# Moving eighteen row scalings from VectorE to GpSimd at the end of an attention and mixture-of-experts kernel

## What is computed

```python
x = attention(q, k, v)                 # 2304 tokens x 512, chunks of 64
h = x @ w_in;  x = (h * clip(h + 3, 0, 6) / 6) @ w_out
noisy_logits = x @ w_gate + log1p(exp(x @ w_noise)) * noise
top2 = ...; top2_w = softmax over the two
out = zeros((2304, 512))
for e in range(8):
    for k in range(2):                 # tokens whose k-th choice is e
        out[mask] += top2_w[mask, k, None] * (relu(x[mask] @ w1[e]) @ w2[e])
```

## Time and profile before

| | us |
|---|---|
| median of three runs | 1018.02 |
| lowest and highest | 1017.66, 1019.82 |
| the profiled execution | 1018.02 |
| its span, first to last instruction | 1016.4 |
| TensorE busy | 988.8 (97%) |
| GpSimd busy | 479.7 (47%) |
| VectorE busy | 444.6 (44%) |
| TensorE's mean granted clock | 0.994 |

### The profile page before, as it was taken

The page is one execution under the profiler, slowest core; times in us unless marked ns, Lnnn a source line. Parts: engine busy times, 40 slices in busy tenths (PEclk is TensorE's granted clock), DMA queues, the critical chain, the costliest instruction groups (busy, mean ns, idle before and its releaser), DMA issues.

```text
span 1016.4 us, 18598 instructions
## 1 busy us (share of the span) xinstructions
PE 988.8 (97%) x5883; PEld 835.9 (82%) x5884; DVE 444.6 (44%) x848; ACT 340.9 (34%) x483; POOL 479.7 (47%) x743
## 2 busy tenths in 40 slices
PE   6999999999999999999999999999999999999997
PEld 6888988987988988988877878878787887888885
DVE  5454355344345445464454443334334333433334
ACT  3333333332343343332422333333333333333332
POOL 5994001100100200597463785848578584934344
PEclk9999999999999999999999999999999999999999
DMA  9832032132123120524366455656656565346629
GB/s 331 305 100 64 18 108 84 46 122 79 49 75 113 63 63 2 219 93 163 105 222 151 125 165 138 187 147 171 171 137 165 141 188 145 87 100 175 166 82 343
DMA packets 119836, 137.39 MB, mean 135 GB/s; under 512 B 80352, under 2 KB 80480, under 8 KB 119776
## 3 DMA queue, kind: packets, MB, share of 16 engines
q1 hardware_dynamic: 95536, 70.79, 24.4%
q0 software_dynamic: 12288, 44.05, 13.6%
q10 hardware_dynamic: 11952, 21.76, 6.9%
HBM read 77.07 MB, written 40.63 MB: 116 GB/s over the span
## 4 chain that ended last, share of the span: by engine, by line
PE 69%; POOL 21%; DVE 3%; issue 3%; DMA 2%; POOLq 1%; ACT 1%; ACTq 0%; SPq 0%; DVEq 0%
PE ps L1231 20%; PE ps L1245 13%; POOL W L490 11%; PE ps L1218 11%; PE ps L1350 11%; POOL W L486 8%; PE ps L1249 6%; PE ps L1267 1%; DMA hT_halves<-h_halves 1%; PE ps L1187 1%; POOL EXraw L473 1%; PE ps L1166 1%; POOLq L465 1%; PE ps L1174 1%; PE ps L1286 1%
## 5 line engine op out<-in xcount | busy, mean ns | idle before, releaser
L1350 PE MATMUL ps<-W,hT_part 128*128 (+1 forms) x1032 | 254.2, 401 | 3.5 <-DVE hT_part L1122 2.2
L1218 PE MATMUL ps<-W,xg_part 128*128 (+1 forms) x1032 | 249.2, 396 | 4.9 <-POOLq L497 4.1
L1218 PEld LDWEIGHTS ps<-W,xg_part 128*128 128x128 f32 x1032 | 192.6, 187 | 53.6 <-issue 7.3
L1350 PEld LDWEIGHTS ps<-W,hT_part 128*128 128x128 f32 x1032 | 193.5, 191 | 46.7 <-issue 4.2
L1231 PE MATMUL ps<-x_part,W 128*128 128x384 f32 x1152 | 224.8, 344 | 2.8 <-issue 2.3
L1231 PEld LDWEIGHTS ps<-x_part,W 128*128 128x128 f32 x1152 | 200.9, 189 | 8.0 <-issue 2.7
L449 POOL DMA_INDIRECT routed_x<-x,slot_blk x36 | 36.5, 1014 | 320.3 <-DVE slot_blk L877 224.9
L490 POOL TENSOR_TENSOR W<-EXraw,W 128x256 fp32r<-128x256 f32 x224 | 164.5, 766 | 4.7
L1245 PE MATMUL ps<-W,g_part 128*128 128x512 f32 x576 | 149.9, 395 | 0.0
L486 POOL TENSOR_SCALAR W<-EXraw 128x256 fp32r<-128x256 f32 x224 | 106.6, 503 | 85.6 <-PE ps L1350 77.9
L1245 PEld LDWEIGHTS ps<-W,g_part 128*128 128x128 f32 x576 | 106.7, 188 | 17.8
(11 more groups left out here) (183 smaller groups left out, 791.3 us busy)
## 6 DMA issues: line engine op xcount, KB each, us to landing
EXraw<-in_w POOLq DMA_DIRECT2D x24, 1024.0 KB, 5.9
QKV<-qkv SPq DMA_DIRECT2D x15, 768.0 KB, 5.5
routed_y<-y_sb ACTq DMA_DIRECT2D x43, 256.0 KB, 4.4
routed_y<-zero_tile SPq DMA_DIRECT2D x14, 768.0 KB, 7.3
xg<-routed_x ACTq DMA_DIRECT2D x40, 256.0 KB, 2.9
Wraw<-w_moe SPq DMA_DIRECT2D x16, 512.0 KB, 9.9
EXraw<-in_w SPq DMA_DIRECT2D x8, 1024.0 KB, 7.3
out<-y_lo SPq DMA_DIRECT2D x18, 256.0 KB, 4.8
```

What stands on the lines that cost most here:

```text
L1218: last = nc.tensor.matmul(dst, a(ha), b(hb), start=(i == 0), stop=(i == n - 1))
L1350: last = nc.tensor.matmul(ps[:, 4, :], hT_part[hh][:, n, :], W[hw][:, weights(slot, W1W + n * DM, DM)], start=(n == 0 and k == 0), stop=(n ...
```

## The change

The 18 multiplications of `y_lo` are taken from VectorE's program and put into GpSimd's, between its 18 gathers into `y_lo` and the wait for the last expert's stores. GpSimd makes the same waits (for the weights, and for all gathers into `y_lo`) before them. The other uses of the semaphore `lo_scaled` stay as they are.

```diff
                 gather(t, 0, y_lo[t][:, :], lo_got[t % ABREAST])
+            pool.wait_ge(wmix_ready, 2)
+            for r in range(ABREAST):
+                pool.wait_ge(lo_got[r], 16 * T // ABREAST)
+            for t in range(T):
+                nc.gpsimd.tensor_scalar(y_lo[t][:], y_lo[t][:], wmix[:, t, 0:1], None, ALU.mult).then_inc(lo_scaled, 1)
+
             done = pool.value_load(done_tab[0:1, E - 1:E], min_val=1, max_val=G)
             pool.wait_ge(y_stored, done * 16)
...
             take_y(GL - 1)
 
 
-            dve.wait_ge(wmix_ready, 2)
-            for r in range(ABREAST):
-                dve.wait_ge(lo_got[r], 16 * T // ABREAST)
-            for t in range(T):
-                nc.vector.tensor_scalar(y_lo[t][:], y_lo[t][:], wmix[:, t, 0:1], None, ALU.mult).then_inc(lo_scaled, 1)
             for t in range(T):
                 dve.wait_ge(lo_scaled, t + 1)
                 dve.wait_ge(hi_got[t], 16)
```

## The result

The change makes the kernel slower. Over 20 executions each the medians are 1022.47 us after and 1015.23 us before; the ratio of the comparison is 1.0076, with a 95% interval from 1.0057 to 1.0094, so about 7.7 us on 1015 (the two medians alone differ by 7.2 us). One execution of before took 1263.72 us, far above all others; it moves that median by under 0.1 us. That lies above the range given (1016.2 to 1019.8) and on the side of the third rival.

The account below looks back on a forecast made before the run. TensorE's chain was taken as the bound, the output chain having 0.57 us of slack: 1012.75 (last store issued) + 2.1 (landing) + 0.85 = 1015.7, + 1.62 = 1017.3 us; range 1016.2 to 1019.8.

Parts of the forecast that it names:

- the third rival: GpSimd becomes the bound: at 1.13 us a scaling or more the gather starts too late; 1027.2 us at 1.53; chance 9%.
- The stall of the first gather: First gather into `y_hi` is held by VectorE's scalings, 5.05 us against 0.95; removing them makes the output chain 4.10 us earlier.
- The price of one scaling: One 128x512 scaling on GpSimd taken at 0.76 us from L486's rows; 18 take 13.7 us and end at 976.5.
- the cover of 15.7 us: GpSimd's idle time from the last `y_lo` gather's landing (962.80) to 978.50, meant to hide the 18 scalings.
- The high end of the bounds: If the weight cost as much as a second input: 1.53 us a scaling, 27.6 us for 18, ending at 990.4.
- The slope: All of L486's 0.38 us for 256 elements grows with length, giving 0.76 us for 512.
- the 2.0 us for the load and the wait: Load of `done_tab` and wait behind GpSimd's scalings: 1.25 and 0.77 us, 2.0 us if both came in full.
- Its rule: The output chain can start 0.57 us later at no cost; beyond that slack, each later us counts one for one.
- The sum of the forecast: TensorE's chain alone sets the end: last `y_sb` store at 1012.75 lands in 2.1 us, giving 1017.3 us, 0.07% below before.
- Rival S: From the experiments: the first gather's stall was paid in before, so freeing it gives 2 to 4 us less; no chance given.
- Its instructions don't move: TensorE's chain keeps its times after the change, so the last store of `y_sb` is still issued at 1012.75.
- The range: Expected time of the changed kernel, 1016.2 to 1019.8 us; the slow rival and the full clock lie outside, 13% together.

Follow-up runs that it names:

- e9: The changed kernel with a second operation (add 0.0) in GpSimd's scalings, timed against the kernel before: ratio 0.9978, 1013.50 us.
- e10: The kernel before with the 18 scalings still on VectorE but ahead of its last `take_y`: ratio 0.9970 to before, 1013.45 us.
- e18: The same kernel as e9, without a limit on gathers, timed on the chip of the limited ones: 1023.24 us, ratio 1.0000 to before.
- e6: The changed kernel with add 0.0 as second operation in each scaling, a first look by trace: 0.67 us a scaling, no kernel time given.
- e11: The kernel of e9 with 18 more GpSimd instructions (times 1.0, add 0.0) behind the scalings: ratio 1.0015 to before, 1.5 us above.

## Why the prediction was wrong

**The stall of the first gather** was read rightly. Without VectorE's scalings beside it, it takes 0.94 to 1.01 us, and the distance from the first to the second gather falls from 5.35 us to 1.24 to 1.32 us. The stores to `out` came 1.9 to 4.5 us earlier than in the first trace of before (the runs without a limit with a start of 3.6), where 4.1 was forecast. The changed kernel has this gain too, and it is worth nothing there.

**The price of one scaling is the step that failed.** The prediction took 0.76 us, "since L486 is the same operation". It measured 1.55, twice that, and the cover of 15.7 us was short by 12 us. The high end of the bounds, 1.53, had the number by luck: it was argued from a second input, and a weight per partition costs only 0.08 us. L486 and the scaling differ in a thing that the bounds didn't name, the number of operations: L486 multiplies by 1.0 and adds 0.0, the scaling only multiplies. The slope, doubling 0.38 to 0.76, was a little high: the form with two operations took 0.67.

**The rival that came** is the third, given 9%. It had the gather at 992.4 - 974.9 = 17.5 us behind the last `take_y`; measured were 15.8, because the 2.0 us for the load and the wait behind the scalings shrank to 0.15 (their wait was over long before). Its rule, shift less 0.57 us of slack, then gives 15.8 - 7.7 - 0.6 = 7.5 us, against about 7.7 measured.

**The sum of the forecast**, the change as it would be with scalings that fit into the cover, was tested by e9, e10 and e18. In the traces of e9 and e10, without a stall and with last matmuls as long as before's, it is right: 0.8 us less, against the 0.7 predicted, and the last store of `y_sb` lands in the forecast 2.1 us in both. (e6, with last matmuls of 8.67 us, ends at 42.0.) The medians gave 2.2, 3.0 and 0 us less, and the part beyond 0.8 is not accounted for piece by piece. One candidate is Rival S in executions with short last matmuls: an estimate from the table is 41.5 - (36.2 + 2.9) = 2.4 us, where 2.9 us is what e9 and e10 have from that store to the end. What the sum lacked is the stall of ScalarE, up to 13 us, which the one trace of before did not have and three later ones had. "Its instructions don't move" was wrong for TensorE's chain.

**The range** was too narrow: it left the third rival out, though one end of the stated bounds led to it, and it was laid around 1018.02, while the medians of before ran from 1015.1 to 1022.6 us over the series of this study.

**The advice against the move.** The Trainium skill ("GPSIMD Engine Reference", section 4.1) says to use VectorE for elementwise work. For the form that was used the runs agree (1.55 us a scaling, 7.7 us lost); with two operations it made no difference (e9 and e10, 1013.50 and 1013.45 us). The size that it gives fits neither form: the Trainium skill ("GPSIMD Engine Reference", section 3.1) has 769 ns for 512 elements of a tight one-input loop, by which, as an estimate, the 18 would have been hidden. The runs show 0.59 and 0.67 us for two operations and 1.46 and 1.55 us for one. On the gather beside VectorE's scalings the Trainium skill ("SBUF — State Buffer", the box on the DVE blocks DMA trap) and the runs agree: 5.05 us beside them, 0.95 us without.

**What stays open** is the origin of ScalarE's stalls. They occurred in 9 of the 13 traces in which the gathers are not limited and start 3.6 or 7.7 us behind the last `take_y` (the rows of the table with y_sb above 38, without e6, where it is the length of the last matmuls). None of the five traces with a start from 10.7 us on has one. Full DMA engines alone don't explain it: e9 has them at 1.00 and 1.01 from 12 to 32 us, and e11 at 0.99 from 22 to 32 us behind the last `take_y`, both without a stall while ScalarE has work there. Whether the fetching of instructions or the recording of the trace itself is in play was not tried, and no run tells these apart.

## What to carry to other kernels

Price an instruction from a row of the very same form: the number of operations in it can matter more than its operands or its length. If work goes to an engine that also issues the next transfers, compare it with the wait in front of them and not with the engine's idle time as a whole. And ahead of moving work between engines, try moving it by one place on the engine where it is: the scalings ahead of the last `take_y` on VectorE free the gather at no cost in GpSimd time. By the program that is safe only for a routing like this one: if all tiles of the last expert were among the last three, VectorE would wait for gathers that wait in turn for this very `take_y`, and the kernel would hang. The best version run here keeps the scalings on GpSimd with two operations and four gathers at a time: 0.79% below before, in one series on one chip.

## What the runs showed of the hardware

- On GpSimd, 18 `tensor_scalar` in a row on 128x512 float32 take 1.46 to 1.55 us each with one operation, and 0.59 to 0.67 us with a second, empty one (add 0.0).
- An indirect gather that starts beside VectorE's 18 scalings in a row ends 0.82 us behind the last of them. A gather that starts while VectorE already runs a single instruction with two inputs in SBUF (L1122, and the sums L1153) ends 0.8 us behind it, or takes its usual 0.95 us where that is longer. Where such an instruction started during the gather, the gather still took 0.94 to 0.96 us, in all 106 cases from 900 us on in the traces.
- With 18 gathers of 256 KB and the stores behind them under way at once, ScalarE stood still in 9 of 13 traces, for up to 13 us with nothing to wait for; a limit of four gathers took the median 8.3 us down on the same chip. The cause is open.
